# Gates applied to the final rows instead of the expert rows, and the routing chain rearranged, in a fused gated-recurrence, top-1 mixture-of-experts and two-layer network kernel

## The reference

```
# 1. gated recurrence, 4 batches x 8 heads, 768 steps, head size 48
state = alpha_t[:, None] * state + outer(k_t, v_t);  y_t = q_t @ state
# 2. y becomes x of 3072 tokens x 384; eight experts, one per token
logits = normalized(x) @ normalized(emb).T / tau
idx    = argmax(logits)
probs  = exp(logits - max);  probs /= probs.sum() + 1e-9
gate   = probs[idx]
out    = gate * (relu(x @ w1[idx]) @ w2[idx])        # 384 -> 1024 -> 384
# 3. second network, 384 -> 2048 -> 384, no bias
h = out @ w_in;  result = max(0.01 * h, h) @ w_out
```

## Time and profile before

| | |
|---|---|
| runs shown | 843.91, 847.55, 848.63 us, median 847.55 |
| the profiled execution's own time | 845.98 us |
| its span, first to last instruction | 844.2 us |
| mean granted TensorE clock | 0.997 |
| busy: PE, PE weight load, DVE, ACT, POOL | 832.2, 750.9, 420.6, 342.4, 184.7 us |
| instructions in the span | 17203 |

### The profile page before, as it was taken

The page is one execution under the profiler, slowest core; times in us unless marked ns, Lnnn a source line. Parts: engine busy times, 40 slices in busy tenths (PEclk is TensorE's granted clock), DMA queues, the critical chain, the costliest instruction groups (busy, mean ns, idle before and its releaser), DMA issues.

```text
span 844.2 us, 17203 instructions
## 1 busy us (share of the span) xinstructions
PE 832.2 (99%) x5554; PEld 750.9 (89%) x5555; DVE 420.6 (50%) x656; ACT 342.4 (41%) x663; POOL 184.7 (22%) x263
## 2 busy tenths in 40 slices
PE   8899999999999999999999999999999999999998
PEld 7788878898999999989998999998999998999997
DVE  7899969726445444446255533533433433443332
ACT  2455547525443444435244333323323333333332
POOL 6566624332322232222220001001001001000100
PEclk9999999999999999999999999999999999999999
DMA  9999861633435152377203201201011000000101
GB/s 217 232 224 222 187 216 45 237 113 133 152 136 187 38 192 96 126 215 165 103 1 40 38 1 37 38 1 37 10 28 38 0 0 27 11 1 1 39 1 37
DMA packets 46678, 76.38 MB, mean 90 GB/s; under 512 B 19239, under 2 KB 36179, under 8 KB 46640
## 3 DMA queue, kind: packets, MB, share of 16 engines
q1 hardware_dynamic: 41232, 61.08, 27.0%
q0 software_dynamic: 5248, 14.80, 5.1%
q10 hardware_dynamic: 160, 0.01, 0.0%
HBM read 61.67 MB, written 15.60 MB: 92 GB/s over the span
## 4 chain that ended last, share of the span: by engine, by line
PE 93%; DVE 2%; DMA 2%; POOL 1%; issue 1%; ACT 0%; SPq 0%; DVEq 0%; POOLq 0%; ACTq 0%
PE bank L1455 24%; PE bank L1490 24%; PE bank L1428 15%; PE bank L1408 15%; PE bank L1419 3%; PE bank L1252 2%; PE bank L1292 2%; DMA qkas<-qka 2%; PE bank L1269 2%; PE bank L1300 1%; PE bank L1395 1%; PE bank L1258 1%; PE bank L1312 1%; POOL kt L558 1%; PE bank L1243 0%
## 5 line engine op out<-in xcount | busy, mean ns | idle before, releaser
L1455 PE MATMUL bank<-yT,wts 128*128 128x512 f32 x864 | 217.0, 395 | 0.0
L1490 PE MATMUL bank<-wts,gs 128*128 128x384 f32 x1152 | 215.0, 335 | 0.0
L1490 PEld LDWEIGHTS bank<-wts,gs 128*128 128x128 f32 x1152 | 202.3, 188 | 8.9 <-issue 0.3
L1455 PEld LDWEIGHTS bank<-yT,wts 128*128 128x128 f32 x864 | 160.8, 188 | 30.6
L1218 DVE TENSOR_TENSOR g<-bank,small 128x512 f32<-128x512 f32 x96 | 66.4, 692 | 172.5 <-ACT small L809 172.5
L1408 PE MATMUL bank<-wts,gxT 128*128 (+1 forms) x558 | 141.6, 398 | 0.6 <-DVE gxT L1092 0.6
L1428 PE MATMUL bank<-wts,hT 128*128 x744 | 137.2, 339 | 0.0
L809 ACT ACTIVATE small<-bank 128x512 f32<-128x512 f32 x96 | 57.5, 599 | 187.6 <-PE bank L1455 184.6
L1428 PEld LDWEIGHTS bank<-wts,hT 128*128 128x128 f32 x744 | 128.5, 188 | 0.2
L1408 PEld LDWEIGHTS bank<-wts,gxT 128*128 128x128 f32 x558 | 102.0, 188 | 19.7 <-issue 0.8
L1220 DVE TENSOR_TENSOR gs<-g,gs 128x512 fp32r<-128x512 f32 x96 | 66.6, 694 | 67.0 <-ACT gs L812 67.0
(11 more groups left out here) (186 smaller groups left out, 735.2 us busy)
## 6 DMA issues: line engine op xcount, KB each, us to landing
raw<-w SPq DMA_DIRECT2D x14, 1536.0 KB, 7.1
qkas<-qka SPq DMA_DIRECT2D x40, 289.5 KB, 5.1
vs<-v SPq DMA_DIRECT2D x24, 192.0 KB, 5.1
x_rows<-xs SPq DMA_DIRECT2D x24, 192.0 KB, 4.3
yl<-y_rows SPq DMA_DIRECT2D x20, 192.0 KB, 4.7
raw<-w_in SPq DMA_DIRECT2D x2, 1536.0 KB, 7.0
raw<-w_out SPq DMA_DIRECT2D x2, 1536.0 KB, 7.1
raw<-w SPq DMA_DIRECT2D x3, 512.0 KB, 4.0
```

The lines of the kernel that those rows point to most:

```text
L1455: m = pe.matmul(gps[f % 2][:, :], wts[:, 0, w_part, n:n + P], yT[:, u, y_part, k], start=(k == 0 and (w_part, y_part) == (0, 0)), stop=(k ...
L1490: m = pe.matmul(ops[tt], gs[:, f % 4, g_part, tt * P:(tt + 1) * P], wts[:, 1, w_part, f * D:(f + 1) * D], start=(f == 0 and (g_part, w_par ...
```

## The change

- **Gates.** slot_gate, gate_hi, gate_lo, the gate matmuls (L1379), ACT's and POOL's gate products and their semaphores go. ys becomes a plain copy of yeps. The gate of each token is made in `gates` (128 x 24 x 4, three columns zero): `shift_logits` runs on DVE in window 1, Exp on ACT in window 1, `make_gates` on DVE in window 2. After the windows ACT stores the gates to a DRAM array token_gates with four DMAs. POOL gathers them for the 20 scattered tiles with 20 indirect DMAs into row_gates, once the token numbers are in. ACT's `o_copy` waits for all 20 and multiplies the output rows by the gate.
- **Choice.** `choose` does tile selection in two parts: the first 20 tiles in step 2 of the recurrence's last chunk, behind `keep_norms`; the last four after the last `sum_logits`. The steps of the row norm are no longer between.
- **Scan.** incl restarts at each expert: the scan multiplies by `fresh` (0 at each expert's first tile, else 1; two POOL memsets in the recurrence's end). The subtractions and copies for counts and starts go.
- **Marks.** win_hot and slot_hot compare with the int32 posi; posf goes. win_val has one part instead of three. ACT multiplies 18 tiles by the token number, POOL the last six in one product.
- **slot_src** is made from tokps by one instruction (subtract, maximum, int32 output), the copy tok behind it. clear and empty move to `place_slots`, and the window-code steps from `differs` on move behind the first low parts of gxT.
- ACT starts the split of expert 0's weights directly after the root. `each_window` is peeled one window pair further on ACT and DVE.
- Fillers: HOT 13 to 5, POS 27 to 22, SLOT 3 to 2, GATE 2 removed, GATHER 3 to 16.

```diff
@@ constants
-        START_BUSY, FILL_BUSY, HOT_BUSY, POS_BUSY, SLOT_BUSY, GATE_BUSY, GATHER_BUSY = 12, 5, 13, 27, 3, 2, 3
+        START_BUSY, FILL_BUSY, HOT_BUSY, POS_BUSY, SLOT_BUSY, GATHER_BUSY = 12, 5, 5, 22, 2, 16
@@ POOL
-                for j, val in vals[0:1 if g >= LO_TILES // SLOT_TILES else 2]:
-                    pool.tensor_tensor(win_val[:, some, j, :], win_hot[:, some],
-                                       val.unsqueeze(2).to_broadcast([P, SLOT_TILES, WC]), ALU.mult).then_inc(gates_placed, 1)
+            pool.memset(fresh[:, :, 0:1], 0.0).then_inc(scan_starts, 1)
+            pool.memset(fresh[:, :, 1:TILES], 1.0).then_inc(scan_starts, 1)
+            some = slice(TILES - SLOT_TILES, TILES)
+            pool.wait_ge(win_marked, 2)
+            pool.tensor_tensor(win_val[:, some], win_hot[:, some],
+                               token1[:, some].unsqueeze(2).to_broadcast([P, SLOT_TILES, WC]), ALU.mult).then_inc(last_placed, 1)
...
             pool.wait_ge(tokens_in, 16)
+            pool.wait_ge(gates_stored, 16 * BATCHES)
+            for n in range(TILES - TG):
+                pool.indirect_dma_start(
+                    out=row_gates[:, n, :], out_offset=None, in_=gate_dram,
+                    in_offset=bass.IndirectOffsetOnAxis(ap=tokens[:, n, 0:1].bitcast(U32), axis=0),
+                    bounds_check=N - 1, oob_is_err=False).then_inc(gates_in, 16)
@@ ACT
-            act.wait_ge(shift_done, 1)
-            act.activation(ex[:, :, :], lg[:, :, :], ACT.Exp).then_inc(exp_done, 1)
             split_hi(act, 0, 0, range(4))
-            for c in range(TILES):
+            for c in range(TILES - SLOT_TILES):
...
-            for c in range(LO_TILES, TILES):
-                act.activation(win_val[:, c, 2, :], win_hot[:, c], ACT.Copy, scale=gate_lo[:, c:c + 1]).then_inc(lo_placed, 1)
...
+                if isinstance(w, int) and w == 1:
+                    act.wait_ge(shift_done, 1)
+                    act.activation(ex[:, :, :], lg[:, :, :], ACT.Exp).then_inc(exp_done, 1)
...
-            each_window(act, step)
+            each_window(act, step, 1)
+            act.wait_ge(gates_made, 2)
+            for b in range(BATCHES):
+                act.dma_start(gate_rows[b], gates[:, b::BATCHES, :]).then_inc(gates_stored, 16)
...
-                act.activation(os_[:, u, tt], ops[tt], ACT.Copy).then_inc(o_copied, 1)
+                n = t * TG + tt
+                if n == 0:
+                    act.wait_ge(gates_in, 16 * (TILES - TG))
+                gate = gates[:, n, 0:1] if t == GROUPS - 1 else row_gates[:, n, 0:1]
+                act.activation(os_[:, u, tt], ops[tt], ACT.Copy, scale=gate).then_inc(o_copied, 1)
@@ DVE
+            def choose(some, n, follow):
+                follow(dve.tensor_tensor(lg[:, some], lgs[:, :].rearrange("p (c e) -> p c e", e=E)[:, some],
+                                         embr[:, :].unsqueeze(1).to_broadcast([P, n, E]), ALU.mult))
+                follow(dve.tensor_reduce(top[:, some], lg[:, some], AX.X, ALU.max))
+                follow(dve.tensor_tensor(cand[:, some], lg[:, some], over(top[:, some]), ALU.is_equal))
+                follow(dve.tensor_tensor(cand[:, some], cand[:, some],
+                                         prio[:, :].unsqueeze(1).to_broadcast([P, n, E]), ALU.mult))
+                follow(dve.tensor_reduce(best[:, some], cand[:, some], AX.X, ALU.max))
+                dve.tensor_tensor(hot[:, some], cand[:, some], over(best[:, some]), ALU.is_equal).then_inc(hot_ready, 1)
...
                 if is_last(c) and b == 2:
                     keep_norms()
+                    dve.wait_ge(norms_kept, 1)
+                    dve.wait_ge(lg_summed, CH - 1)
+                    choose(slice(0, TILES - BATCHES), TILES - BATCHES, link)
...
+            choose(slice(TILES - BATCHES, TILES), BATCHES, follow)
+            dve.wait_ge(scan_starts, 2)
             dve.wait_ge(rank_sums, 1)
-            start("main", dve.tensor_tensor_scan(flat(incl[:, :, :]), totps, zeros[:, :], 0.0, ALU.add, ALU.add))
+            start("main", dve.tensor_tensor_scan(flat(incl[:, :, :]), flat(fresh[:, :, :]), totps, 0.0, ALU.mult, ALU.add))
...
-            start("main", dve.tensor_copy(posf[:, :, :], posi[:, 1:3, :]))
...
-                                  spread(posf[:, 1, some], P), ALU.is_equal).then_inc(slots_hot, 1)
+                                  spread(posi[:, 2, some], P), ALU.is_equal).then_inc(slots_hot, 1)
+            dve.wait_ge(sq_done, TILES)
...
+            dve.tensor_scalar(slot_src[:, :], tokps[:, 0:W], 1.0, 0.0, ALU.subtract, ALU.max).then_inc(tables_ready, 1)
             start("side", dve.tensor_copy(tok, tokps[:, 0:W]))
-            after("side")
-            start("side", dve.tensor_scalar(clear, tok, 1.0, 0.0, ALU.subtract, ALU.max))
-            after("side")
-            dve.tensor_copy(slot_src[:, :], clear).then_inc(tables_ready, 1)
...
+                if isinstance(w, int) and w == 1:
+                    shift_logits()
+                if isinstance(w, int) and w == 2:
+                    make_gates()
...
-                dve.tensor_scalar(ys[:, u, 0:D], yeps, slot_gate[:, ds(w, 1)], None, ALU.mult).then_inc(ys_ready, 1)
-            each_window(dve, step, 1)
+                dve.tensor_copy(ys[:, u, 0:D], yeps).then_inc(ys_ready, 1)
+            each_window(dve, step, 2)
@@ PE
-            pe.wait_ge(hot_ready, 1)
+            pe.wait_ge(hot_ready, 2)
...
-                if c % 2 == 0:
+                if c == TILES - SLOT_TILES:
+                    pe.wait_ge(last_placed, 1)
+                elif c < TILES - SLOT_TILES and c % 2 == 0:
                     pe.wait_ge(tokens_placed, c + 2)
...
-                m = pe.matmul(gateps, slot_hot[:, c, :], flat(win_val[:, c, 1:3]), start=(c == 0), stop=(c == TILES - 1))
-            m.then_inc(gates_summed, 1)
```

More of the change, by code:

```diff
@@ L943, in _ @@
             root, safe, rec, mean, scale = (nrm[:, j, :] for j in (0, 1, 2, 3, 4))
-            top, total, best, gate = (red[:, j, :] for j in range(4))
-            starts, counts, wins, cum, base, cx = (exp8[:, j, :] for j in range(6))
+            wins, cum, base, cx = (exp8[:, j, :] for j in range(4))
             dve.wait_ge(lg_summed, CH)
-            dve.wait_ge(norms_kept, 1)
-            start("main", dve.tensor_tensor(lg[:, :, :], lgs[:, :].rearrange("p (c e) -> p c e", e=E),
-                                            embr[:, :].unsqueeze(1).to_broadcast([P, TILES, E]), ALU.mult))
@@ L970, in _ @@
-            dve.tensor_tensor(hot[:, :, :], cand[:, :, :], over(best, E), ALU.is_equal).then_inc(hot_ready, 1)
-            after("side")
-            start("side", dve.tensor_scalar(mean, mean, 0.5, 1e-6, ALU.mult, ALU.add))
-            start("main", dve.tensor_tensor(lg[:, :, :], lg[:, :, :], over(top, E), ALU.subtract))
-            after("side")
-            start("side", dve.reciprocal(scale, mean))
-            after("main")
-            dve.wait_ge(rank_sums, 1)
-            start("main", dve.tensor_tensor_scan(flat(incl[:, :, :]), totps, zeros[:, :], 0.0, ALU.add, ALU.add))
@@ L991, in _ @@
+            start("main", dve.tensor_scalar(wins, incl[:, :, TILES - 1], 1.0 / P, (P - 1.0) / (2 * P), ALU.mult, ALU.add))
             dve.wait_ge(rank_sums, 2)
@@ L1015, in _ @@
                                             base.unsqueeze(2).to_broadcast([P, E, TILES]), ALU.add))
-            after("side")
-            start("side", dve.tensor_tensor(gate_lo[:, :], gate, gate_hi[:, :].bitcast(F32), ALU.subtract))
             after("main")
@@ L1107, in _ @@
             split_lo(dve, 0, 0, range(3, 4))
-            kept, kept_sum, kept_from, back, limit, back_by, limit_by = (exp_early[:, j, :] for j in range(7))
-            start("main", dve.tensor_tensor(kept, incl[:, :, TILES - TG - 1], starts, ALU.subtract))
-            after("main")
+            kept = incl[:, :, TILES - TG - 1]
+            kept_sum, kept_from, back, limit, back_by, limit_by = (exp_early[:, j, :] for j in range(6))
             start("main", dve.tensor_tensor_scan(kept_sum, kept, zeros[:, 0:E], 0.0, ALU.add, ALU.add))
```

158 lines of the change are left out of this document (69 added, 89 removed).

## The result

The changed kernel takes 850.48 us (median of 11 runs, 846.3 to 854.08) where the kernel before takes 844.82 us (11 runs on the same chip): a ratio of 1.0059, 95% interval 1.0038 to 1.0080. It was forecast at 842.8 us, with faster a little more likely than no change; it is slower. The profiled execution took 848.84 us with a span of 847.1 us, 2.9 us more than the span before.

What follows compares the result with a forecast made beforehand. It took the matrix engine to bound the windows and second network, leaving routing before the first expert matmul to shorten. 1.84 + 0.87 + 0.87 + 0.44 = 4.02 us, 842.0 from the profiled 845.98; forecast 842.8, range 839.8 to 846.4.

Steps and rivals of the forecast that it cites:

- Part 1, the choice: One-hot tile choice on DVE after the recurrence: 20 tiles chosen earlier for free, four left, hot ends 122.90; gain 1.84 us.
- Part 2: Routing from scan start to window marks: fewer small DVE steps, 4.86 us becomes 3.99; gain 0.87 us.
- Part 3: Routing from window marks to the read of tokps: 6.84 us becomes 5.97, set by ACT's path; gain 0.87 us.
- no full block: DVE's slot_hot beside POOL's product: they hinder each other without fully blocking; a full wait would cut the gain by 0.1.
- Part 4: slot_src made by one instruction from PSUM, POOL's issue and the gather's landing unchanged; gain 0.44 us.
- mixed types: Rival: comparing with int32 in marks and slot_hot halves the rate and costs 4.0 us, giving 846.8; chance 0.04.
- So they don't bind: PE's 16 fillers behind the sums end at 137.7, before the gather lands at 138.6, so they don't delay hidden(0).
- The clock falls: Rival: PE's idle stretches in routing drop the granted clock, losing 1.65 us if at hidden(0), giving 844.4; chance 0.08.
- Moved work: Gate work moved to the windows, gate stores, POOL's gathers and scaled output copies all fit in slack; cost 0.
- POOL's 20 small gathers: Gate gathers after the windows, 1.28 us each, done at 475 while the first output copy comes at 511; cost 0.
- the gates come late: Rival: ACT's first output copy waits for gathers slower than 3.1 us each; 850.8 at 3.5; chance 0.05 with the like.
- Scaling the output by a column instead of a constant keeps ACT's one pass: ACT's output copies in the second network: still one pass when scaled by the gate column; cost 0.

Runs made afterwards that it cites:

- split copies: The changed kernel with four gathers ahead of each group's scatters and two of a group's four output copies made by DVE: 841.82 us, ratio 0.9952.
- two bursts: The changed kernel with ten gathers up front and ten after the first group's output scatters: 843.57 us, ratio 0.9977.
- fourteen: The changed kernel with 14 gathers up front and six after the first group's output scatters: 843.22 us, ratio 0.9975.
- split with one pause: The changed kernel with two of a group's four output copies on DVE, all 20 gathers up front and one wait after the tenth: 842.38 us, ratio 0.9956.
- no gathers: The changed kernel without the 20 gate gathers and ACT's wait for them, early tiles scaled by the gates column: 843.37 us, ratio 0.9967.
- 28: The changed kernel with 28 gathers of 32 rows in a row in place of 20 of 128: 861.37 us, ratio 1.0198.
- forty: The changed kernel with 40 gathers of 32 rows in a row in place of 20 of 128: 878.65 us, ratio 1.0393.
- plain copies: The changed kernel with output copies not multiplied by the gates, the gathers kept: 848.11 us, ratio 1.0026.
- late burst: The changed kernel with all 20 gathers held back by one wait on g_hi, so that they ran from 461.5 us: 855.76 us, ratio 1.0118.
- quarter version: The changed kernel with 20 gathers of 32 rows each in place of 128: 841.89 us, ratio 0.9957.

## Why the prediction was wrong

**Part 1, the choice** came as worked out: hot ends at 122.00, 1.64 us behind lgs, where the kernel before took 3.49; 1.85 against 1.84. **Part 2:** scan to marks 127.06 - 123.09 = 3.97, forecast 3.99. **Part 3:** marks to the read of the sums 133.17 - 127.06 = 6.11, forecast 5.97, so a gain of 0.73 in place of 0.87. That this came so near is in part luck, since not ACT's path set the end but PE's own queue: from 128.59, when the first slot_hot was there, its four groups of token matmuls and the twelve fillers between them (0.54 us for four) follow without idle to 133.15, and ACT's copies had ended at 131.57, the last slot_hot at 131.87. The last two slot_hot took 2.13 together, 0.3 us more than two alone, as assumed.

But that this is no full block, as the prediction says, is a wrong reading. The third slot_hot ended at 130.69, GpSimd's product 0.37 later at 131.06, the fourth slot_hot 0.81 after that at 131.87. In the kernel before, with five such products in a row, each ended 0.36 or 0.37 us after the DVE instruction beside it, and each DVE instruction a fixed time after the product: 0.82 with 768 columns, 0.42 with 384, 0.27 with 248. The two take strict turns. The Trainium skill (SBUF — State Buffer, Who interferes with whom) has it so: the two share a port under an exclusive lock. The trace agrees; the price was right because 0.36 of the product's 0.68 us is all that is left to wait for.

**Part 4** and the landing came within 0.15 us. The sum was 4.02, and 3.96 were measured. The **mixed types** rival is out: 0.95 us for 768 columns compared with int32, and 0.95 before.

**The clock** held at 1.00 through the routing of this execution, but this was luck. Sixteen of the traces have the changed routing. In six of them the granted clock fell to 0.50 somewhere between 131 and 143 us; in the three with the old routing it did not. Where it fell for 6.8 us (split copies, two bursts, fourteen, split with one pause), the routing took 20.6 us and not 18.6. The 16 fillers behind the sums and their windows, after and in the split copies:

```profile
132.98 3.90 PE L1254 MATMUL bank<-wts 128*128 128x512 f32 x16
```
```profile
132.79 6.28 PE L1274 MATMUL bank<-wts 128*128 128x512 f32 x16
```
```profile
133.00:138.00 5.00, 4.07 (x20) 3.07 (x20) 4.19 (x7) 0.47 (x1) 3.13 (x3) 1.00 0.14 39
```
```profile
133.00:138.00 5.00, 5.00 (x13) 3.90 (x14) 4.18 (x7) 0.00 (x0) 3.13 (x3) 0.51 0.14 39
```

At the lower clock the fillers end 1.4 us after the gather's landing (an estimate: issue at 134.24 and the 3.4 us of the other traces) and hold PE themselves; the prediction has "So they don't bind". So the rival *The clock falls*, which had a chance of 0.08, is real: half of the gain in routing goes where it strikes. In five of the six PE was busy the whole of the eight microseconds before the fall, as it was in the changed kernel's trace, which kept the clock; what tips it is open. In the sixth (no gathers) it fell at 142.5 us, at hidden(0), and the expert windows took 1.3 us more than in the changed kernel.

**The step that failed is "Moved work", and in it the sentence on "POOL's 20 small gathers", with its "All at 0".** In place of 0 the runs show a stall of PE, ACT and DVE that cost 5.9 us in the profiled execution and 7.8 us in the medians, 0.9%: it goes with the gathers (ratio 0.9967) or with one pause among them (0.9971), and comes with them into the kernel before (1.0152). What it said of the gathers themselves is close: 1.37 us apart on average (1.28 forecast), over at 473.7 us (475), some 37 us ahead of need. It asked only whether they come in time. The rival *the gates come late* asked the same and gave them a price only above 3.1 us each. Neither asked what a long burst does to engines that have nothing to do with it, and the rows before had no burst to read it from: the longest run of output scatters without a wait in that trace is four, the four tiles of a group. Nothing "by the nearest rows" could price it; what the prediction should have done is to say that no row shows 20 in a row, and keep a bound above zero for it. With that the chance of slower could not have been 0.05.

The same step had a second, small failure: "Scaling the output by a column instead of a constant keeps ACT's one pass." It does, but the pass takes 582 ns in place of 492, and four of them stand on PE's path in every group. The wait that would have told it is in the trace before as 0.28 us on the weight loads; a stretch with PE at 100% hides it. Taking the scale away gave back 1.5 us by the trace.

The account in the profiled executions: -0.88 (recurrence, by chance) -3.96 (routing) +0.24 (the expert windows) +5.9 (stall) +1.5 (copies) = +2.8, measured +2.9. In the medians the change is 5.0 us (by the ratio) to 5.7 us slower, and this execution's stall was probably one of the shorter ones: its 848.84 us lies below the median of 850.48, and without the gathers the median falls by 7.8 us (1.0059 - 0.9967, of 845). The start of the sum was off too: the three times shown have a median of 847.55, all eleven one of 844.82, so 842.8 stood for a gain of 4.8 us and would have been one of 2.0.

## What to carry to other kernels

Work that is moved onto an idle engine and "done in time" can still cost time while it runs: look for a stretch in which several engines stand idle at once with nothing named as late, and ask what runs on the engine that goes on. Break a long run of GpSimd's indirect DMAs with a wait for their own landing, here one after ten; it cost nothing (the first group took 66.40 us) and gave back 0.9%. Look at the granted clock in more than one execution before calling a clock rival settled. And before adding to an operation in front of the bounding engine, look at the weight loads' waits, not only at the busy share.

## What the runs showed of the hardware

- A run of indirect DMAs that GpSimd issued without a pause, 1.2 to 1.6 us apart, made PE, ACT and DVE stall until after the burst: PE's last late matmul came 2.0 us after the end of the last gather in the changed kernel, 4.2 us with 28 and 7.0 us with forty. The stall began with about the 17th where the burst started at 446 us, with the 14th or 15th in the plain copies, and with the 12th or 13th (476.9 us) in the late burst, so it is not a fixed count. Fourteen were free, and so were 20 with a pause of 2.0 us after the tenth or at 1.86 us on average. In the stall of forty, PE's matmuls start at multiples of 0.70 us (2.10, 1.43, 2.10 us apart), in that of twenty every 0.7 us.
- It isn't the bandwidth of the DMA engines. Their share was 0.07 in the stall of the changed kernel, 0.01 with forty, and the gathers' packets came at their usual rate, 32 for each gather whether it had 32, 64 or 128 rows. The Trainium skill (DMA: Bandwidth & Descriptors, Queues, rings and completion order) has each DMA engine serve its queues in turn, a packet at a time; by that alone a burst could delay others only on busy engines, and these were nearly idle.
- Open is what fills up. That it takes 16 to 24 us to show, outlasts the burst and holds three engines at once would fit a delayed supply of instructions. Against it: the 16 KB packets of the instruction queue q8 come at 461.1 and 485.8 us with one pause, where nothing stalls, and at 462.4 and 493.0 in the changed kernel, later by the stall, and none is under way in it. Not excluded is that the recording of the profile has a part: each execution here has a recorded span and clock, and none was timed without. Nor was a long run of another GpSimd instruction tried, or one of plain DMAs. Open too is why 20 gathers of 32 rows are free: up to the 17th they run as the first 17 of forty, which stall there. They had two longer ones among them (1.78 and 1.41 us), so a chance pause may have begun the count anew, but 28 of 32 rows stalled with one as long as the first (1.85 us), and all six times of the quarter version lie between 841.02 and 842.78 us.
- GpSimd's two-input product and DVE's two-input comparisons take strict turns, with the times given under part 3.
- The granted clock fell to 0.50 in six of sixteen traces of the same routing, and not in the other ten.
- A copy of 128x384 from PSUM takes ACT 0.582 us with a column as scale and 0.492 us without, and DVE 0.612 us and 0.557 us.
